# Pooled attention, two dense products and routed experts: 512 tokens at a time instead of 288

## The reference, cut to what matters

```python
def reference(q, k, v, w1, w2, w3, w_out, modality_id, w_gate, bias, e_w1, e_w2):
    k_p, v_p = mean of k, v over groups of 8 rows          # 576 -> 72 keys
    x = softmax(q @ k_p.T / 8) @ v_p                        # per batch and head
    x = x.transpose(0, 2, 1, 3).reshape(4608, 512)
    a, b = x @ w1, x @ w2                                   # (4608, 1024) each
    x2 = ((a * b) @ w3) @ w_out                             # (4608, 512)
    e = argmax(x2 @ w_gate + bias[modality_id])             # one of 8 experts
    out = softmax weight of e * (relu(x2 @ e_w1[e]) @ e_w2[e])
```

## Time and profile before

| | |
|---|---|
| median of 3 runs | 1235.84 us (1235.25 to 1237.42) |
| the profiled execution's own time | 1237.33 us |
| its span, first to last instruction | 1235.4 us |
| mean granted TensorE clock | 0.991 of full |
| start, until the first product | 85.2 us |
| batches, products and tiles | 85.2 to 779.0 us |
| expert steps | 779.0 to 1235.4 us |
| VectorE busy, ScalarE busy, GpSimd busy | 43%, 22%, 17% |

### The profile page before, as it was taken

The page is one execution under the profiler, slowest core; times in us unless marked ns, Lnnn a source line. Parts: engine busy times, 40 slices in busy tenths (PEclk is TensorE's granted clock), DMA queues, the critical chain, the costliest instruction groups (busy, mean ns, idle before and its releaser), DMA issues.

```text
span 1235.4 us, 29802 instructions
## 1 busy us (share of the span) xinstructions
PE 1203.9 (97%) x12148; PEld 1136.3 (92%) x12149; DVE 528.1 (43%) x1276; ACT 271.4 (22%) x625; POOL 211.2 (17%) x247
## 2 busy tenths in 40 slices
PE   7999999999999999999999999999999999999995
PEld 5888899999999999999999999989999899899894
DVE  0745546536557456456364143622222233222221
ACT  1322222312322212223122123211111131111110
POOL 2560102111221022021020000022122112121120
PEclk9999899999999999999999999999999999999998
DMA  9641222123023032032130005134111111111111
GB/s 359 202 154 29 82 70 68 75 72 107 32 85 108 28 91 95 28 93 82 45 85 5 32 1 180 35 106 151 35 48 54 34 34 53 34 51 51 34 52 34
DMA packets 41249, 93.02 MB, mean 75 GB/s; under 512 B 9395, under 2 KB 16691, under 8 KB 40116
## 3 DMA queue, kind: packets, MB, share of 16 engines
q1 hardware_dynamic: 32292, 66.68, 16.1%
q0 software_dynamic: 6400, 20.50, 5.2%
q10 hardware_dynamic: 2448, 4.26, 1.0%
HBM read 70.93 MB, written 21.01 MB: 74 GB/s over the span
## 4 chain that ended last, share of the span: by engine, by line
PE 96%; DMA 1%; DVE 1%; issue 1%; ACT 0%; SPq 0%; POOL 0%; POOLq 0%; DVEq 0%
PE ab L726 17%; PE ab L727 17%; PE ab L728 17%; PE rt L726 6%; PE x2p L726 6%; PE rt L727 5%; PE x2p L727 5%; PE x2p L728 5%; PE rt L728 5%; PE sct L790 3%; PE ab L739 2%; PE ab L812 2%; PE sct L871 1%; PE rt L739 1%; PE x2p L739 1%; DMA wo_x<-in_moe_w_out 1%
## 5 line engine op out<-in xcount | busy, mean ns | idle before, releaser
L726 PE MATMUL ab<-xth,e1h 128*128 128x256 f32 x608 | 170.2, 280 | 2.1 <-DVE xtl L1401 2.1
L727 PE MATMUL ab<-xtl,e1h 128*128 128x256 f32 x608 | 171.3, 282 | 0.0
L728 PE MATMUL ab<-xth,e1l 128*128 128x256 f32 x608 | 170.0, 280 | 0.0
L726 PE MATMUL ab<-xh,w1h 128*128 128x288 f32 x512 | 154.2, 301 | 6.4 <-DVE pb L1214 2.8
L726 PE MATMUL ab<-xh,w2h 128*128 128x288 f32 x512 | 151.4, 296 | 0.0
L727 PE MATMUL ab<-xl,w2h 128*128 128x288 f32 x512 | 151.4, 296 | 0.0
L728 PE MATMUL ab<-xh,w2l 128*128 128x288 f32 x512 | 151.2, 295 | 0.0
L727 PE MATMUL ab<-xl,w1h 128*128 128x288 f32 x512 | 151.0, 295 | 0.0
L728 PE MATMUL ab<-xh,w1l 128*128 128x288 f32 x512 | 150.9, 295 | 0.0
L1250 DVE TENSOR_TENSOR ac<-ab,ac 128x288 f32<-128x288 f32 x128 | 58.4, 456 | 193.1 <-ACT ac L1054 191.4
L1054 ACT ACTIVATE ac<-ab 128x288 f32<-128x288 f32 x128 | 52.6, 411 | 337.9 <-PE ab L728 332.7
(11 more groups left out here) (195 smaller groups left out, 2548.6 us busy)
## 6 DMA issues: line engine op xcount, KB each, us to landing
kv<-in_v SPq DMA_DIRECT2D x24, 512.0 KB, 4.8
qt<-in_q SPq DMA_DIRECT2D x8, 1280.0 KB, 5.9
kv<-in_k SPq DMA_DIRECT2D x16, 576.0 KB, 7.7
x_rows<-xr SPq DMA_DIRECT2D x36, 256.0 KB, 3.3
stage<-in_moe_w SPq DMA_DIRECT2D x8, 1024.0 KB, 13.4
vp<-v_rows SPq DMA_DIRECT2D x32, 192.0 KB, 3.5
w3b<-in_moe_w ACTq DMA_DIRECT2D x16, 256.0 KB, 6.3
wo_x<-in_moe_w_out SPq DMA_DIRECT2D x8, 256.0 KB, 7.2
```

What stands on the lines that cost most here:

```text
L726: pe.matmul(outp, lh, rh, start=first, stop=False)
L727: pe.matmul(outp, lh, rl, start=False, stop=False)
L728: return pe.matmul(outp, ll, rh, start=False, stop=last)
```

## The change

The tokens of a batch are taken as 512 and 64. Each of the 8 batches is one stage of 512 tokens (`MAIN`), J = 8 rounds of 24 matmuls 512 wide, and 4 tiles. The 64 left over of each batch are put, as the attention is made, into `x_tail`; after the eighth batch they are a ninth stage of 512 tokens. The nine stages are written out on every engine, without loops. The tables of what is laid between are rewritten for 8 rounds, and a score step's wait now stands right ahead of it, behind the round's matmuls. The first tile of a stage waits for `gh` and `gl` of 7 rounds ahead of its first matmul and for those of the eighth ahead of its last block. The expert steps are as they were.

```diff
-HS = S // 2
+STAGES = B + 1
+MAIN = N // STAGES
+G = MAIN // P
+TAIL = S - MAIN
+GT = TAIL // G
-J = 2 * FC
+J = FC
-FIRST_SCORE = {2: 0, 5: 1, 8: 2, 10: 3, 13: 4}
-LATER_SCORE = {0: 2, 4: 3, 9: 4}
...
-ONEHOT_AT = {8: (0, 1), 9: (2, 3), 13: (4,)}
-TABLE_AT = {9: (0, 1), 10: (2, 3), 14: (4,)}
+FIRST_SCORE = {1: 0, 3: 1, 4: 2, 5: 3, 6: 4}
+LATER_SCORE = {0: 2, 2: 3, 4: 4}
+FIRST_PART = {1: [(0, 0)], 2: [(1, 0), (2, 0)], 3: [(0, 1)], 4: [(1, 1), (2, 1), (0, 2)], 5: [(1, 2), (2, 2), (0, 3)],
+              6: [(1, 3), (2, 3), (0, 4)], 7: [(1, 4), (2, 4)]}
+LATER_PART = {0: [(0, 2)], 1: [(1, 2), (2, 2)], 2: [(0, 3)], 3: [(1, 3), (2, 3)], 4: [(0, 4)], 5: [(1, 4), (2, 4)]}
+ONEHOT_AT = {4: (0, 1), 5: (2, 3)}
+TABLE_AT = {5: (0, 1), 6: (2, 3)}
...
             def a_b(b, j):
-                cols = slice(HS * half, HS * (half + 1))
-                fs = slice(f * P, (f + 1) * P)
-                for n, (wh, wl) in enumerate(((w1h, w1l), (w2h, w2l))):
-                    for c in range(KC):
-                        mm = split(bank[:, n, 0:HS], wh[:, c, fs], wl[:, c, fs], xh[:, c, cols],
-                                   xl[:, c, cols], c == 0, c == KC - 1)
+                for cs in (range(0, 2), range(2, 4)):
+                    if j == 0 and cs[0]:
+                        x_split(8 * (b + 1) if b < B else 8 * b + KC)
+                    for n, (wh, wl) in enumerate(((w1h, w1l), (w2h, w2l))):
+                        for c in cs:
+                            mm = split(bank[:, n, :], wh[:, c, fs], wl[:, c, fs], xh[:, c, :], xl[:, c, :],
+                                       c == 0, c == KC - 1)
                 mm.then_inc(ab_done, 1)
...
+            def mul_x2(b, g, part):
...
                 for f in range(FC):
+                    if g == 0 and part == 0 and f in (0, FC - 1):
+                        pe.wait_ge(gh_ready, J * b + (J if f else J - 1))
+                        pe.wait_ge(gl_ready, J * b + (J if f else J - 1))
...
+            def products(b, rounds):
                 for j in range(J):
+                    a_b(b, j)
+                    if b and j == 1:
+                        rank(b - 1)
+                    for g in TABLE_AT.get(j, ()) if b else ():
+                        table(b - 1, g)
                     if j in rounds:
                         may_score(b + 1, rounds[j])
                         score(rounds[j])
...
+            for b in range(STAGES):
+                products(b, FIRST_SCORE if b == 0 else LATER_SCORE if b + 1 < B else {})
...
+                slots(b)
...
             def hi_x(b, part):
...
                 for g in range(4):
+                    if g % 2 == 0:
+                        to = x_tail[:, cs, tail_cols(b, g // 2)].rearrange("p n (g t) -> p n g t", t=GT)
+                        act.activation(to, tail_bank(g // 2), ACT.Copy, scale=1.0 / POOL)
+            def hi_tail():
+                act.wait_ge(ab_done, J * B)
+                for c in range(KC):
+                    act.activation(xh[:, c, :], x_tail[:, c, :], ACT.Copy).then_inc(xh_ready, 1)
...
+            def lo_tail():
+                for c in range(KC):
+                    dve.wait_ge(xh_ready, 8 * B + c + 1)
+                    dve.tensor_tensor(xl[:, c, :], x_tail[:, c, :], xh[:, c, :].bitcast(F32),
+                                      ALU.subtract).then_inc(xl_ready, 1)
...
+            def products(b, parts):
                 for j in range(J):
                     mul_ab(b, j)
                     if j:
+                        lo_g(b, j - 1)
+                    if b and j == 0:
+                        route_pick(b - 1)
                     for part, m in parts.get(j, ()):
                         soft[part](b + 1, m)
+                    if b and j == 1:
+                        route_gate(b - 1)
+                    if b and j == 2:
+                        route_rank(b - 1)
+                    for g in ONEHOT_AT.get(j, ()) if b else ():
+                        route_onehot(b - 1, g)
+                    if j == 6:
+                        route_bias(b)
+                    if b and j == 7:
+                        route_add(b - 1)
+                    if b == B and j == 3:
                         first_expert()
+                    if b == B and j == 7:
                         first_rows()
+                lo_g(b, J - 1)
```

More of the change, by code:

```diff
@@ L450, in load_k @@
             def load_k(b, m):
-                if not (isinstance(b, int) and b == 0):
+                if b:
                     sp.wait_ge(v_out[2 - m], 16 * b)
@@ L537, in load_piece, with move_stage @@
                              src.rearrange("e p c f -> p (e c) f")).then_inc(stage_in[c], 16)
[L539 to L565, removed]
+            def move_stage(b):
+                if b:
+                    store_meta(b - 1)
+                if b + 2 < B:
+                    bring_qk(b + 2)
+                if b == B:
+                    sp.wait_ge(first_ready, 1)
+                    e = sp.value_load(first_i[0:1, 0:1], min_val=0, max_val=E - 1)
+                    sp.wait_ge(ab_done, J * STAGES)
+                    for c in range(4):
+                        load_piece(e, c)
+                for g in range(G):
+                    t = G * b + g
+                    sp.wait_ge(xr_ready, 2 * (t + 1))
+                    sp.dma_start(x_rows[P * t:P * (t + 1), 0:DM], xr[:, g % 2, 0:DM]).then_inc(x_stored[g % 2], 16)
+                if b + 2 < B:
+                    bring_v(b + 2)
+            for b in range(STAGES):
+                move_stage(b)
+            store_meta(B)
             sp.wait_ge(runs_ready, 1)
@@ L828, in a_b @@
[L828 to L842 removed]
+                fs = slice(j * P, (j + 1) * P)
@@ L843, in mul_x2 @@
+                mm.then_inc(ab_done, 1)
+            def mul_x2(b, g, part):
+                t, col = G * b + g, P * g
+                if t or part:
                     pe.wait_ge(xr_ready, 2 * t + part - 1)
-                if part and not (isinstance(b, int) and b == 0):
+                if part and b:
                     pe.wait_ge(acc_added, b)
@@ L986, in after_h @@
                 if f == 4:
[L987 removed]
+                    rank(B)
                 if f == 7:
[L989 removed]
+                    table(B, 0)
             def after_y(f):
[L992 to L993 removed]
+                if f < G - 1:
+                    table(B, f + 1)
             mul_h(0, 1, after_h)
@@ L1140, in hi_piece @@
                                stage[:, c, :], ACT.Copy).then_inc(hi_split[c], 1)
-            def pair(i, first, last):
-                products(i, 0, None if first else (i - 1, 1), FIRST_PART if first else LATER_PART)
-                slots(i, 0, True, not last)
-                products(i, 1, (i, 0), {} if last else LATER_PART)
-                slots(i, 1, not last, not last, (lambda c: hi_piece(1, c)) if last else None)
-            pair(0, True, False)
-            with act.Fori(1, B // 2 - 1) as i:
-                pair(i, False, False)
-            last = B // 2 - 1
-            pair(last, False, True)
+            for b in range(STAGES):
+                products(b, FIRST_PART if b == 0 else LATER_PART if b + 1 < B else {})
+                slots(b)
             def hi_ht(t):
@@ L1410, in lo_xt, with slots @@
                 ins.then_inc(meta_copied, 1)
-            def slots(i, par, pv, att, extra=None):
-                b = batch(i, par)
+            def slots(b):
+                pv, att = b + 1 < B, b + 2 < B
+                if b == B - 1:
+                    lo_tail()
                 if pv:
@@ L1437, in slots, with products @@
                     soft_turn(b + 2, 1)
-                take_logits(i, par, 3)
-                if extra:
-                    extra(3)
-                if not pv:
+                if b < B:
+                    take_logits(b, 3)
+                else:
+                    lo_piece(1, 3)
                     lo_xt(0, 0, 1, None)
-            def products(i, par, before_it, parts):
-                b = batch(i, par)
-                G = tiles_of(before_it[1]) if before_it else 0
+            def products(b, parts):
                 for j in range(J):
```

417 lines of the change are left out of this document (165 added, 252 removed).

## The result

The changed kernel takes 1263.01 us (median of 4 runs, 1261.43 to 1268.76), the kernel before, on the same chip, 1235.55 (1234.07 to 1237.42). The ratio is 1.023, with a 95% interval of 1.0195 to 1.0265: slower, by more than four times what was forecast, and 7 us above the upper end of the range. The profiled execution took 1263.13 us with a span of 1261.3, where before's had 1235.4. So 25.9 us of span are to be found.

What follows compares the result with a forecast made beforehand. The prediction took TensorE, busy 97% of the span, to bound the kernel. Its terms (-16 + 20.3 + 0.3 - 4.7 + 4 - 2.2 + 3.5 + 0.2) gave +5.4, with a clock share +6: 1242 us, range 1233 to 1256.

Steps and rivals of the forecast that it cites:

- start: Ahead of the products: one extra copy into `x_tail` stands in the open, +0.2 us.
- 1, rounds: Product matmuls on TensorE: fewer, wider ones pay the fixed price per matmul less often, -16 us.
- 2, stage ends: End of each stage's products: first tile waits for the last rounds' chain, 2.26 us nine times, +20.3; ninth stage +0.3.
- 3, first stage: First stage: old waits and lowered clock of 8.3 us go, smaller new ones come, -4.7 us.
- 4, one-hot rows: Round 5 of stages 1 to 6: VectorE's one-hot rows come late for table matmuls, +4 us (0 to 7).
- 5, loop: TensorE's wait where its loop turns back goes in the written-out code, -2.2 us.
- 6, last tiles: turn, store: Before the experts: uncovered turn of rows +5.3, store wait -1.0, earlier second gather -0.8; sum +3.5 us.
- a share of one clock fall: Lowered TensorE clock beyond the first stage: raises the summed +5.4 us to +6.
- the rival of the clock: Clock falls at 5 to 9 stage ends, 1.7 us each, 8 to 15 us more: 1250 to 1257; chance 0.15.
- the earlier gather of the second step: Expert steps: one table less lets the second step's gather start 0.8 us earlier, -0.8 us.

Runs made afterwards that it cites:

- the run: The kernel before with its loops over the stages written out, nothing else changed: 1233.69 us, ratio 0.9976 to before.
- one-hot alone: The changed kernel with one-hot rows and table matmuls of stages 1 to 6 one round earlier: 1247.52 us.
- GpSimd alone: The changed kernel with GpSimd's key sums held until the stage's table matmuls are through: 1248.52 us.
- the filler: 18 useless matmuls 260 wide ahead of each stage's first tile, added to the changed kernel with one-hot rows a round earlier: 1247.74 us.

## Why the prediction was wrong

The sign was right and the size wrong: +6 forecast, +26 to +27 measured. First the span: start -1.3 (forecast +0.2), from first product to first expert product 693.9 to 723.9 = +30.0, what follows -2.8; together +25.9. By the steps of the forecast:

| step | forecast | measured |
|---|---|---|
| 1, rounds | -16 | -15.4 (72 x 5.44 for 128 x 3.18) |
| 2, stage ends | +20.3, +0.3 | +20.9 (9 x 2.32) |
| 3, first stage | -4.7 | -5.2 |
| 4, one-hot rows | +4 | +12.5 |
| 5, loop | -2.2 | -2.3; -2.7 by the run |
| 6, last tiles: turn, store | +5.3, -1.0 | +5.2, about -1.0 |
| clock, beyond step 3 | a share of one fall, under 1 | 8 falls at 1.5: +12 |
| what is laid between the rounds | no term | +2.8 |

- **Parts 1, 2, 5 and 6** held, each within a microsecond. The wide matmul costs what the expert's did, and the chain's length out of single durations was 2.54 against 2.49 (2.26 and the spacing of 0.23). In the first stage it was 0.9 that the block of round 7 waited, not 1.9, and the clock fell there as assumed. Two sums are off by a tenth, which decides nothing: 5.9 - 0.8 + 0.1 is 5.2, and the chain of part 4 adds up to 5.7.
- **Part 4 failed in its size**: "GpSimd's sums ... cost the chain 0.7 and the one-hot rows something too. I take 0.8 in five stages". The "something" was the main part. I had priced `ohr` and `ohc` at 0.54 a pair from a row without GpSimd beside it, though the same rows showed what GpSimd does to its neighbours. Beside it the first pair takes 2.0 and the second 0.9 (stage 3), and the tables wait 1.3, 3.3, 2.7, 2.6 and 2.7 us in stages 1 to 5, 12.5 in all. The upper bound of 7 was too tight too. The run that holds GpSimd back shows the cause.
- **The clock failed with it, and cost as much**: the sum held "a share of one clock fall", and eight more than in part 3 came, 12 us. I had taken the stall of 2.1 us at the loop's jump as nearest, with its 1.00, against the one of 2.82. The earlier trace rows have a third, 2.07 us at 150.87, and the clock of its stretch in the earlier trace rows is 0.95: it fell there too. So two of the three rows spoke for a fall, and I had weighed one of them. Five of nine stage ends were followed by a fall, and four of the five stages with a wait at the tables (stage 1, where the two waits are 0.5 and 0.3, had none), which the rival of the clock didn't count as it had only the stage ends. Its price of 1.7 each was near the 1.5 measured. With the rule of the Trainium skill cited there (TensorE: Matmul & The Clock Gate, section on queue depth-cycling: short idle times between groups make the clock swing) the trace agrees. With part 4 at 12.5 the rival's 1250 to 1257 becomes 1259 to 1266, and holds the 1263. The experts' part has one fall in both kernels.
- A term was missing: what is laid between the rounds is dearer when the rounds are wide. Three score steps cost 54.60 - 51.58 = 3.0 us before and 50.03 - 46.54 = 3.5 after (stage 6 less stage 7): +2.8 in six stages. With the products 256 wide, in the same schedule, it is 3.0 again.
- Of the experts' -2.8 some 0.9 is the earlier gather of the second step (0.8 forecast). The other 2.0 lie behind the last matmul, 13.4 us before and 11.4 after. That stretch takes 11.4 to 13.6 in the twelve profiled executions, so it says nothing of the change.

The measured column sums to 29.5, against 30.0 from first product to first expert product. What stays open is why the clock falls behind one stall of 2.16 us and not behind the next one like it: what went before it in the same stage doesn't sort them (stage 2 had a fall at its tables and one at its end, stage 3 only the first).

## What to carry to other kernels

A longer round in a software pipeline costs twice: the chain behind the last round grows and there is less other work to lay on it. Let the consumer ask block by block, and do the blocks that are ready of all its parts first. Price a VectorE operation from a row with the same neighbour on GpSimd as it will have, and count a stall of 2 us on a busy TensorE at its length and about one more us for the clock (here nine falls of 1.5 behind thirteen stalls of about 2 us).

## What was not expected of the hardware

- Small one-hot operations grow to 2.4 to 3.8 times their length beside GpSimd (0.28 to 1.07, 0.42 to 1.03), a `TENSOR_SCALAR` of 128x8 from 0.17 to between 0.47 and 1.20, while the transpose on VectorE keeps its 0.78.
- Stalls of 2.16 us of the same form led to a lowered clock in five of nine cases in each of three kernels (after, one-hot alone, GpSimd alone), at other stages in each, and in eight of nine with the products 256 wide; with the filler in them in none of the stage ends 1 to 8.
- A matmul with 256 columns took 120 ns in the products and 117 in the experts; in the products what is above the columns is 13 to 14 for 256, 288 and 512.
- The first product starts between 83.8 and 86.5 us in kernels whose start is the same: 2 to 3 us of a single execution's span say nothing of a change.
